# Layer one's nonlinearity: one ScalarE function from PSUM in place of tanh and a VectorE gate

## What is computed

```python
def _attn_ref(q, k, v, tau):
    qn = q / (norm(q, axis=1) + 1e-06); kn = k / (norm(k, axis=1) + 1e-06)
    a = softmax(kn.transpose(0, 2, 1) @ qn / tau)      # 256 x 256
    return v @ a

def _moe_ref(x, w_in, w_out):                          # "layer one"
    h = x @ w_in
    g = h * (1.0 / (1.0 + np.exp(-1.702 * h)))
    return g @ w_out

def _moe2_ref(x, w_in, w_out):                         # "layer two"
    h = x @ w_in
    g = np.where(h > 0.0, h, np.exp(np.minimum(h, 0.0)) - 1.0)
    return g @ w_out
```

## Time and profile before

| | |
|---|---|
| median of 3 runs (lowest, highest) | 1067.88 us (1066.73, 1068.07) |
| the profiled execution, and its span | 1067.18 us, 1065.3 us |
| PE busy | 1036.0 us, 97% of the span |
| DVE busy | 880.6 us, 83% |
| ACT busy | 771.9 us, 72% |
| POOL busy | 61.5 us, 6% |
| mean granted TensorE clock | 0.993 of full speed |
| DMA | 46.27 MB |

### The profile page before, as it was taken

The page is one execution under the profiler, slowest core; times in us unless marked ns, Lnnn a source line. Parts: engine busy times, 40 slices in busy tenths (PEclk is TensorE's granted clock), DMA queues, the critical chain, the costliest instruction groups (busy, mean ns, idle before and its releaser), DMA issues.

```text
span 1065.3 us, 14446 instructions
## 1 busy us (share of the span) xinstructions
PE 1036.0 (97%) x4614; PEld 859.8 (81%) x4614; DVE 880.6 (83%) x1398; ACT 771.9 (72%) x1366; POOL 61.5 (6%) x54
## 2 busy tenths in 40 slices
PE   9879999999999999999998999999999999999996
PEld 8767778888888888888886787887888888888896
DVE  7889987888878888787998888888887887888775
ACT  7676766666666666566678788888788788888874
POOL 0042300000000000000323000000000000000000
PEclk9989999999999999999999999999999999999999
DMA  9933002002102102003113001201101110210112
GB/s 311 273 78 60 1 1 65 15 1 60 20 1 60 18 1 57 1 1 119 41 40 114 1 1 40 40 1 40 28 12 41 20 21 3 53 21 1 21 21 35
DMA packets 113531, 46.27 MB, mean 43 GB/s; under 512 B 98992, under 2 KB 104112, under 8 KB 112816
## 3 DMA queue, kind: packets, MB, share of 16 engines
q1 hardware_dynamic: 113456, 45.36, 16.1%
HBM read 33.03 MB, written 12.32 MB: 43 GB/s over the span
## 4 chain that ended last, share of the span: by engine, by line
PE 83%; DVE 7%; issue 4%; ACT 4%; SPq 1%; DMA 0%; DVEq 0%; ACTq 0%
PE bank L923 27%; PE bank L925 27%; PE bank L924 27%; DVE gated L823 2%; PE bank L936 1%; ACT xo L601 1%; DVE g_lo L836 1%; DVE blk_lo L760 1%; ACT act_out L571 1%; DVE sumsq L672 1%; ACT blk_hi L473 1%; ACT g_hi L589 0%; DVE bank L814 0%; DVE t_sum L755 0%; SPq L282 0%
## 5 line engine op out<-in xcount | busy, mean ns | idle before, releaser
L923 PE MATMUL bank<-g_hi,w_dn_hi 128*128 128x512 f32 (+1 forms) x768 | 296.5, 386 | 0.6 <-DVE g_lo L836 0.6
L924 PE MATMUL bank<-g_lo,w_dn_hi 128*128 128x512 f32 (+1 forms) x768 | 296.1, 386 | 0.0
L925 PE MATMUL bank<-g_hi,w_dn_lo 128*128 128x512 f32 (+1 forms) x768 | 296.0, 385 | 0.0
L923 PE MATMUL bank<-blk_hi,w_up_hi 128*128 128x512 f32 (+1 forms) x672 | 263.7, 392 | 13.7 <-ACT u L511 6.1
L836 DVE TENSOR_TENSOR g_lo<-gated,g_hi 128x512 fp32r<-128x512 f32 (+1 forms) x384 | 261.2, 680 | 16.7 <-ACT g_hi L589 8.4
L924 PE MATMUL bank<-blk_lo,w_up_hi 128*128 128x512 f32 (+1 forms) x672 | 259.7, 386 | 0.0
L925 PE MATMUL bank<-blk_hi,w_up_lo 128*128 128x512 f32 (+1 forms) x672 | 259.6, 386 | 0.0
L589 ACT CAST g_hi<-gated 128x512 fp32r<-128x512 f32 (+1 forms) x288 | 175.7, 610 | 88.9 <-DVE gated L823 84.3
L823 DVE SCALAR_TENSOR_TENSOR gated<-act_out,bank 128x512 f32<-128x512 f32 (+1 forms) x288 | 192.3, 668 | 0.8 <-ACT act_out L567 0.7
L923 PEld LDWEIGHTS bank<-blk_hi,w_up_hi 128*128 128x128 f32 x672 | 126.5, 188 | 51.7 <-ACT u L511 9.5
L923 PEld LDWEIGHTS bank<-g_hi,w_dn_hi 128*128 128x128 f32 x768 | 144.5, 188 | 28.5 <-DVE g_lo L836 1.3
(11 more groups left out here) (112 smaller groups left out, 847.3 us busy)
## 6 DMA issues: line engine op xcount, KB each, us to landing
qk<-in_q_dram SPq DMA_DIRECT2D x15, 384.0 KB, 3.7
qk<-in_k_dram SPq DMA_DIRECT2D x15, 384.0 KB, 5.3
x_scratch<-xo SPq DMA_DIRECT2D x10, 512.0 KB, 3.1
raw<-x_scratch SPq DMA_DIRECT2D x5, 1024.0 KB, 5.1
out_dram<-blocks SPq DMA_DIRECT2D x40, 128.0 KB, 2.7
blocks<-in_v_dram SPq DMA_DIRECT2D x36, 128.0 KB, 3.2
stage<-in_moe_w_in_dram SPq DMA_DIRECT2D x8, 512.0 KB, 8.4
stage<-in_moe_w_out_dram SPq DMA_DIRECT2D x8, 512.0 KB, 4.8
```

What stands on the lines that cost most here:

```text
L923: nc.tensor.matmul(out_ps, w_hi, x_hi, start=start, stop=False, skip_group_check=goes_on)
L924: nc.tensor.matmul(out_ps, w_hi, x_lo, start=False, stop=False, skip_group_check=goes_on)
L925: return nc.tensor.matmul(out_ps, w_lo, x_hi, start=False, stop=stop, skip_group_check=goes_on)
```

## The change

In layer one ACT applies one function, `Gelu_apprx_sigmoid`, to h, and writes it into `gated` directly. It stands at the place of the tanh. The gate on DVE goes for U < 48; a block's readiness is then told by `c_act` and no longer by `c_gate` (`wait_gated`). Since ACT now writes `gated`, it is ACT that waits for `g_lo` of two blocks before (`c_glo`), the reader of the buffer that it overwrites. The factor 0.5 at L601 becomes 1.0. Layer two is as before, apart from the waits of its first two blocks.

```diff
+        def wait_gated(engine, n):
+            if n < block_of(LAYER, 0):
+                engine.wait_ge(c_act, n + 1)
+            else:
+                engine.wait_ge(c_gate, n - block_of(LAYER, 0) + 1)
...
             def gelu(U, x):
                 h_ready(U, x)
-                nc.scalar.activation(act_at(U, x), h_of(U, x), ACT.Tanh, scale=GELU_ALPHA / 2).then_inc(c_act, 1)
+                if block_of(U, x) >= 2:
+                    act.wait_ge(c_glo, block_of(U, x) - 1)
+                nc.scalar.activation(gated[:, x % 2, 0:width(pair_of(U))], h_of(U, x),
+                                     ACT.Gelu_apprx_sigmoid).then_inc(c_act, 1)
...
             def g_hi(U, x):
                 n, w = block_of(U, x), width(pair_of(U))
-                act.wait_ge(c_gate, n + 1)
+                wait_gated(act, n)
...
                 if U:
                     g_lo(U - 1, H21)
-                    gate(U - 1, H12)
+                    if U > LAYER:
+                        elu(U - 1, H12)
                     g_hi(U - 1, H12)
-                if U < ALL:
-                    gate(U, H11)
+                if LAYER <= U < ALL:
+                    elu(U, H11)
```

More of the change, by code:

```diff
@@ L13 @@
 BANK = 512
-GELU_ALPHA = 1.702
 A11, A12, A22, S1, S2, S3, S4 = range(7)
@@ L558, in h_ready @@
                     act.wait_ge({H11: c_h11, H22: c_h22, H12: c_h12}[x], U + 1)
-                if block_of(U, x) >= 2:
-                    act.wait_ge(c_gate, block_of(U, x) - 1)
             def act_at(U, x):
@@ L566, in gelu @@
                 h_ready(U, x)
-                nc.scalar.activation(act_at(U, x), h_of(U, x), ACT.Tanh, scale=GELU_ALPHA / 2).then_inc(c_act, 1)
+                if block_of(U, x) >= 2:
+                    act.wait_ge(c_glo, block_of(U, x) - 1)
+                nc.scalar.activation(gated[:, x % 2, 0:width(pair_of(U))], h_of(U, x),
+                                     ACT.Gelu_apprx_sigmoid).then_inc(c_act, 1)
             def elu_first(U, x):
                 h_ready(U, x)
+                if block_of(U, x) >= block_of(LAYER, 2):
+                    wait_gated(act, block_of(U, x) - 2)
                 nc.scalar.activation(act_at(U, x), h_of(U, x), ACT.Relu, scale=-1.0).then_inc(c_relu, 1)
@@ L601, in evacuate @@
                     nc.scalar.mul(xo[:, d, tile, 0:w], acc[tile][d][:, 0:w],
-                                  0.5 if s < NP else 1.0).then_inc(c_evac, 1)
+                                  1.0).then_inc(c_evac, 1)
             def side(U):
@@ L806, in sum22_of @@
                 if U:
-                    dve.wait_ge(c_gate, block_of(U - 1, H22) + 1)
+                    wait_gated(dve, block_of(U - 1, H22))
                 nc.vector.tensor_tensor(h22[:, 0:w], u3[:, 0:w], sum2212[:, 0:w], ALU.add).then_inc(c_h22, 1)
@@ L814, in sum12_of, with elu @@
                 nc.vector.tensor_tensor(sum2212[:, 0:w], u2[:, 0:w], sum2212[:, 0:w], ALU.add).then_inc(c_h12, 1)
-            def gate(U, x):
+            def elu(U, x):
                 n, w = block_of(U, x), width(pair_of(U))
@@ L819, in gate @@
                 dve.wait_ge(c_act, n + 1)
-                if n >= 2:
-                    dve.wait_ge(c_glo, n - 1)
-                ops = (ALU.add, ALU.mult) if U < LAYER else (ALU.subtract, ALU.max)
+                dve.wait_ge(c_glo, n - 1)
                 nc.vector.scalar_tensor_tensor(out=gated[:, n % 2, 0:w], in0=act_out[:, n % 2, 0:w], scalar=1.0,
-                                               in1=h, op0=ops[0], op1=ops[1]).then_inc(c_gate, 1)
+                                               in1=h, op0=ALU.subtract, op1=ALU.max).then_inc(c_gate, 1)
             def g_hi(U, x):
                 n, w = block_of(U, x), width(pair_of(U))
-                dve.wait_ge(c_gate, n + 1)
+                wait_gated(dve, n)
                 if n >= 4:
@@ L890, in unit @@
                     sum12_of(U - 1)
-                    gate(U - 1, H21)
+                    if U > LAYER:
+                        elu(U - 1, H21)
                     g_lo(U - 1, H22)
@@ L908, in unit @@
                 weights(U)
-                gate(U, H22)
+                if U >= LAYER:
+                    elu(U, H22)
             for U in range(ALL + 1):
@@ L1006, in product1 @@
                 if U >= 2:
-                    pe.wait_ge(c_gate, block_of(U - 2, H21) + 1)
+                    wait_gated(pe, block_of(U - 2, H21))
                 product(U, 1, chain[U % 2], A11, X11, True)
@@ L1011, in product2 @@
                 if U:
-                    pe.wait_ge(c_gate, block_of(U - 1, H11) + 1)
+                    wait_gated(pe, block_of(U - 1, H11))
                 product(U, 2, sum11, A12, X21, True)
@@ L1020, in product5 @@
                 if U:
-                    pe.wait_ge(c_gate, block_of(U - 1, H12) + 1)
+                    wait_gated(pe, block_of(U - 1, H12))
                 product(U, 5, sum2212, S1, T1, True)
```

## The result

| | before | after |
|---|---|---|
| median | 1067.97 us (4 runs) | 1059.49 us (4 runs, 1058.55 to 1060.29) |
| ratio to before, 95% interval | | 0.9922 [0.9905, 0.9939] |
| profiled execution, its span | 1067.18, 1065.3 us | 1059.76, 1058.0 us |
| PE busy | 1036.0 us, 97% | 1033.8 us, 98% |
| DVE busy | 880.6 us, 83% | 771.9 us, 73% |

The change saves 8.5 us, 0.8%, and the interval stays clear of 1. The forecast was 1060.2, a gain of 7.7.

What follows compares the result with a forecast made beforehand. PE was taken to be the bound, with 11.9 us of waits to win past the start; less 1.7 and 2.2 left lost and 0.3 for the first load, 7.7 us gained: 1060.2 us, range 1057.5 to 1063.8.

Steps and rivals of the forecast that it cites:

- The sum: Whole kernel: 11.9 us of PE waits, less 1.7 left, 2.2 in unit 48, 0.3 at the start: 7.7 gained.
- split units: Units in which weights are split, one at a time; PE's waits there and in unit 48 were put at 11.9 us.
- B: Weight-splitting unit near 114 us: 1.55 us lost before, 0.5 forecast to stay, at product 7.
- F: Weight-splitting unit near 544 us: 1.9 us lost before, 0.3 forecast to stay with its restart.
- D: Weight-splitting unit near 523 us: 1.9 us lost before, 0.9 forecast to stay, at product 7 with restarts.
- C: Weight-splitting unit near 136 us: 1.55 us lost before, 0 forecast to stay, with g_lo(H22) held up by POOL.
- The first load: ACT's first table load, at layer one's start: 1.28 us, mostly paid by the gate's 0.69; loss 0.3 us.
- rival 1: Each table load costs twice its row, at the start and unit 48: gain 5.1, 1062.8 us; chance 0.10.
- Rival 2: POOL holds up sum12 and both g_lo, about 1.1 us each, in five units: gain 3.2, 1064.7 us; chance 0.09.
- rival 3: Of the 3.9 us left lost, only the load's 1.3 stays: gain 10.3, 1057.6 us; chance 0.10.
- rival 4: ACT's new function is slow: 1069.2 us at 1.2 us each, 1099 at 1.5; chance 0.04.
- Rival 5: Waiting for `c_glo` puts ACT behind DVE as the gate did: within 2 us of before, 1066.5; chance 0.05.

Runs made afterwards that it cites:

- the third run: Changed kernel with an operation of the gate's kind put back on VectorE at each old gate place in layer one, nobody waiting for it: 1071.12 us, ratio 1.0035.
- the second pair: Profiles of both kernels run once more, unchanged: the changed kernel 1059.93 us (ratio 0.9934), the kernel before 1067.55 us (1.0002).

## Why the prediction was right, point by point

- **What bounds it.** Right: 222 matmuls in 50 us in the undisturbed units, with DVE at 41, at 31 and, in the third run, at 41 again.
- **The sum.** From product 3 of unit 0 to the end of the span the two profiles of before take 989.8 and 988.3, those of after 980.4 and 980.8. Without the half-clock matmuls that is 987.0 and 986.7 against 979.0 and 979.2: 7.8 us. The forecast for this stretch was 11.9 - 1.7 - 2.2 = 8.0. The whole spans differ by 7.3 in the first pair of profiles and by 8.4 in the second, the medians by 8.5 in the first round and by 7.6 in the second. That the first pair comes so near 7.7 is partly luck: the changed kernel's profile lost 1.8 us before product 3, apart from the load, and won 1.4 in the half-clock stretch, and neither belongs to the change.
- **What stays in the split units.** Forecast 0.5, 0, 0.9, 0 and 0.3 in B to F, measured 0.12 + 0.27, 0, 0.78, 0 and 0.24. The chain behind it (four VectorE operations, the function, copy_u2) was right for product 7, and the experiment with copy_u2 first took its waits away. In unit 4 (B) one sees it: the function for H11 waits for g_lo until 115.07, and copy_u2 follows:

```profile
115.07 0.60 ACT L573 ACTIVATE gated<-bank 128x512 f32<-128x512 f32 x1 [0.60 <-DVE g_lo L843]
115.57 0.58 ACT L524 COPY u<-bank 128x512 f32<-128x512 f32 x1
```

- **A wait that was left out.** The prediction named as a sign of being wrong that a product waits for g_lo, and one does: of D's 0.78 us, 0.47 are down H22's wait for g_lo(H22) at 519.94, and B's 0.12 are of the same kind. Its own numbers had it: in D g_lo(H22) is ready at 521.72 + 0.53 + 0.61 = 522.9, and down H22 is due three matmuls after product 6, at 521.95 + 0.61 = 522.6. The total for D came out all the same, since PE, once late, waits that much less at product 7. In that unit the sum was right and the place half wrong.
- **POOL's hold on VectorE.** I let g_lo be held and sum12 not. That was right in C (g_lo 1.19 at 132.73), F (1.18 at 537.19) and unit 48 (1.19). For sum12 the row that I gave did not show it: at 135.16 POOL's work had ended at 134.69. In the trace of before, the sum12 at 113.13 would have been the right one, with 0.68 beside POOL's work from 112.68 to 114.48. The page "SBUF — State Buffer", section "SBUF: two separate sides" of the Trainium skill, says why: VectorE and GpSimd share a pair of ports under an exclusive lock, and a VectorE operation with both inputs in SBUF needs it against a GpSimd operation that reads SBUF. The trace agrees: 0.62 with a bank as an input, 1.19 with two SBUF tiles, beside the same work on POOL, which reads two SBUF tiles.
- **The first load.** Forecast loss 0.3, measured 3.98 - 3.70 = 0.28, and 3.98 - 3.66 = 0.32 in the second pair.
- **Unit 48, the term that was mis-sized.** I expected 3.35 us lost to become 2.2, a gain of 1.15. It became 1.74 + 0.69 = 2.4 and, in the second pair of profiles, 2.9 became 2.5: a gain of 0.4 to 0.9. On the side of after the chain through the load was right to 0.2 (product 7 lost 1.74, forecast 1.9), but product 4 lost 0.69 and not 0.3. On the side of before, what I had taken for fixed is the wait of product 4, 1.05 in one profile and 0.55 in the other; one profiled execution was too little there. The sum also left out product 5 of unit 49, which waits for a gate: 0.43 and 0.56 in the two profiles of before, 0.67 and 0.52 after. With it counted the gain is 0.7 and 0.4.
- **DVE's relief** was 109 us, not the 130 that I gave: 192 gates of 0.68 went, but the page has VectorE busy 108.7 us less. In the gates' group the durations overlap with the next instruction's by some 0.08 each (starts 0.60 apart), and busy time doesn't count that twice: 160 x 0.60 and, at 448 columns, 32 x 0.53 make 113. Of the rest, g_lo takes 3.1 us more (261.2 became 264.3), probably since it is now g_lo that is held beside POOL.
- **A slip in the working.** Product 5 restarts a second time in all six units A to F, and not in five; the sum of 11.9 has all six, and the two profiles of before bear it out.
- **The rivals.** The loads at twice their row (rival 1) fall to the rows: the loads at 73.70 and 558.46 follow at once, and the functions behind them too. Rival 2, the wait that moves, has POOL hold up sum12 as well, and that falls to sum12's 0.62 at 555.48; waits did move, but only 1.4 of the 11.9 us, and more of them only where VectorE had its work back or unit 48 another order. That nothing is left (rival 3) needed the start's and copy_u2's new order. The slow function (rival 4) falls to 599 ns. Rival 5, no gain at all, falls to the ratio and to the product 6 waits that are gone.

## What to carry to other kernels

Work taken from an engine that isn't the bound is worth only what it shortens where that engine is late: here 109 us of VectorE's time bought 8 us, all in seven units of 96. With work of the same length put back in the same places, though nobody waited for it, the gain was gone. Find these places by the distance between matmuls, price each by its bracket and the restart behind it, and then walk the queue to what is late next, for every product that follows and not only for the one that waited. A one-line move at the start of a layer (h22 ahead of a chain that it doesn't need) was worth 2 to 3.5 us more (ratio 0.9901 against the changed kernel's 0.9922 and 0.9934), and a look at who waits for whom in the first unit is cheap.

## What was not expected of the hardware

- After the 3.1 to 4.7 us in which PE waits for product 3 (ten profiles) its granted clock falls to half (1.2 of 2.4 GHz; 0.50 from 76.5 to 80 us in the first profile of before: 0.43 us from matmul to matmul in place of 0.23), but not always at once. In six of the ten it was at half from the first matmul on (the restart's row is 0.79 to 0.80 long). In four the restart's row is 0.50, and the clock fell only 0.6 to 1.5 us after PE had begun again. It stayed low for 5 to 12 matmuls, with no tie to the kernel: the program before had 12 and 7, the changed one 5 and 7. Where the wait was 0.80 to 0.94 us (four profiles) it didn't fall there. In unit 48 it fell once, behind two waits of 1.17 and 1.55 us whose restarts are 2.4 us apart. It did not fall behind the changed kernel's 1.47 and 0.45, and not behind the 1.38 and 1.47, restarts 3.6 us apart, of the kernel with VectorE's work put back. What decides it stays open.
- A matmul that restarts after a wait takes 0.34 us to the next one in place of 0.227 (0.31 in place of 0.203 at 448 columns), also when the wait was too short for the profile to show one. With 512 columns there is a shorter kind as well: product 4's restarts, such as the one at 564.15, have rows of 0.47 and take 0.30 to 0.31.
